# A fused attention, token-mixing and channel-mixing kernel: when the helper engines prepare the first weight pair, the Fourier folds and the side blocks

## The reference, cut to what matters

```python
# 1 attention with decay, blocks of 64, 2 batches x 8 heads, 768 x 64
intra = ((qb @ kb.T) * Dmask) @ vb;  inter = (qb * lam_pow) @ kv_state
out[:, :, sl] = intra + inter
kv_state = lam_block * kv_state + (kb * rev_pow).T @ vb
# 2 token mixing and a channel MLP, x: (2, 768, 512)
h  = np.maximum(x.T @ w_tok1, 0) @ w_tok2      # (512,768) @ (768,256) @ (256,768)
u  = x + h.T
x  = u + np.maximum(u @ w_ch1, 0) @ w_ch2      # 512 -> 1536 -> 512
# 3 real part of a 2-D Fourier transform, layer norm, a second MLP
u  = x + np.real(np.fft.fft(np.fft.fft(x, axis=1), axis=2))
un = (u - mean(u)) / np.sqrt(var(u) + 1e-6)
out = u + np.maximum(un @ w_ch1, 0) @ w_ch2    # 512 -> 2048 -> 512
```

## Time and profile before

| | |
|---|---|
| median of 3 runs (lowest, highest) | 600.6 us (599.02, 600.6) |
| the profiled execution, and its span | 599.33 us, 597.5 us |
| PE busy | 576.2 us, 96% of the span |
| DVE, ACT, POOL busy | 360.2, 263.0, 264.7 us (60%, 44%, 44%) |
| chain that ended last | PE 73%, DVE 10%, POOL 8%, ACT 3%, issue 3% |
| mean granted TensorE clock | 0.997 |

### The profile page before, as it was taken

How to read it: one execution, slowest core, us unless ns; L and a number is a source line. 1 busy time by engine, 2 the same in 40 slices (tenths; PEclk the granted TensorE clock), 3 DMA queues, 4 the chain that set the end, 5 groups by cost and what they waited for, 6 DMA issues and landing times.

```text
span 597.5 us, 9160 instructions
## 1 busy us (share of the span) xinstructions
PE 576.2 (96%) x3344; PEld 512.3 (86%) x3344; DVE 360.2 (60%) x675; ACT 263.0 (44%) x558; POOL 264.7 (44%) x306
## 2 busy tenths in 40 slices
PE   8999998899999989999989899999999999999997
PEld 6999886788889877989878779898888989999996
DVE  7887656657654587347786873477765544333323
ACT  6666134455643444333544443335453444443330
POOL 6884116555553473214457732044555233333311
PEclk9999999899999999999999999999999999999999
DMA  8791210322222101101121011021222211212242
GB/s 304 280 351 30 70 36 1 111 92 90 89 70 71 63 27 70 55 19 71 54 71 63 27 71 54 18 71 54 71 71 71 70 62 62 58 53 68 71 141 106
DMA packets 24125, 49.09 MB, mean 82 GB/s; under 512 B 2572, under 2 KB 3472, under 8 KB 24080
## 3 DMA queue, kind: packets, MB, share of 16 engines
q1 hardware_dynamic: 23360, 46.69, 23.6%
q0 software_dynamic: 576, 1.72, 1.0%
q10 hardware_dynamic: 144, 0.10, 0.1%
HBM read 45.35 MB, written 3.15 MB: 81 GB/s over the span
## 4 chain that ended last, share of the span: by engine, by line
PE 73%; DVE 10%; POOL 8%; ACT 3%; issue 3%; DMA 1%; SPq 1%; DVEq 0%; ACTq 0%; POOLq 0%
PE banks L1106 12%; PE banks L1107 11%; PE banks L1108 11%; PE banks L1333 9%; PE banks L1336 9%; PE banks L1335 9%; PE banks L1170 4%; DVE al L707 2%; POOL raw L346 2%; POOL tl L346 2%; PE banks L1130 2%; PE banks L1164 2%; POOL w2l L346 1%; DVE u L914 1%; DVE sums L707 1%
## 5 line engine op out<-in xcount | busy, mean ns | idle before, releaser
L346 POOL TENSOR_TENSOR w2l<-raw,w2h 128x512 fp32r<-128x512 f32 x56 | 77.4, 1383 | 178.4 <-ACT w2h L451 178.4
L1333 PE MATMUL banks<-th,al 128*128 128x384 f32 x392 | 132.9, 339 | 7.9 <-DVE snap L1028 5.0
L1335 PE MATMUL banks<-tl,ah 128*128 128x384 f32 x392 | 132.6, 338 | 0.0
L1336 PE MATMUL banks<-th,ah 128*128 128x384 f32 x392 | 132.4, 338 | 0.0
L451 ACT ACTIVATE snap<-banks 128x384 f32<-128x384 f32 x84 | 41.2, 490 | 133.4 <-PE banks L1336 133.3
L1028 DVE TENSOR_TENSOR snap<-banks,snap 128x384 f32<-128x384 f32 x84 | 46.3, 552 | 75.0 <-PE banks L1336 74.6
L1333 PEld LDWEIGHTS banks<-th,al 128*128 128x128 f32 x392 | 73.9, 189 | 17.5 <-DVE snap L1028 6.2
L707 DVE TENSOR_TENSOR al<-raw,ah 128x512 fp32r<-128x512 f32 (+1 forms) x112 | 83.5, 767 | 8.0 <-ACT ah L451 6.9
L1335 PEld LDWEIGHTS banks<-tl,ah 128*128 128x128 f32 x392 | 73.9, 189 | 6.0
L1336 PEld LDWEIGHTS banks<-th,ah 128*128 128x128 f32 x392 | 73.9, 189 | 0.0
L815 DVE SCALAR_TENSOR_TENSOR h0l<-snap,h0h 128x384 fp32r<-128x384 f32 x56 | 33.7, 602 | 63.7 <-ACT h0h L641 63.6
(11 more groups left out here) (176 smaller groups left out, 947.9 us busy)
## 6 DMA issues: line engine op xcount, KB each, us to landing
raw<-w1b_dram SPq DMA_DIRECT2D x16, 512.0 KB, 3.3
raw<-w2b_dram SPq DMA_DIRECT2D x32, 256.0 KB, 3.0
raw<-w1a_dram SPq DMA_DIRECT2D x12, 512.0 KB, 3.5
raw<-w2a_dram SPq DMA_DIRECT2D x24, 256.0 KB, 3.5
kTs<-kT_dram SPq DMA_DIRECT2D x8, 384.0 KB, 6.0
qTs<-qT_dram SPq DMA_DIRECT2D x8, 384.0 KB, 6.8
kns<-kn_dram SPq DMA_DIRECT2D x8, 384.0 KB, 7.3
vns<-vn_dram SPq DMA_DIRECT2D x8, 384.0 KB, 4.7
```

The lines of the kernel that those rows point to most:

```text
L346: return nc.gpsimd.tensor_tensor(o, i0, i1, ALU.subtract)
L1333: mm(o[:, 0:HALF], al[:, a, cols], th[b][:, t, k, :], start=start and k == 0, stop=False, skip_group_check=True)
L1335: mm(o[:, 0:HALF], ah[:, a, cols], tl[b][:, t, k, :], start=False, stop=False, skip_group_check=True)
L1336: last = mm(o[:, 0:HALF], ah[:, a, cols], th[b][:, t, k, :], start=False, stop=(k == 1), skip_group_check=True)
```

## The change

PE's and SP's instruction lists stay as they are. No instruction is added to or taken from the arithmetic; what changes is the order on ACT, DVE and POOL.

1. Token mixing. ACT makes the high parts of pair 0's weights after the second of the four `gh` tiles, not after the fourth; DVE makes their low parts after the second `gl`. POOL makes the combinations of pair 1 right after the down weights of pair 0, before the block sums' low parts (`tl`), and the clearing and loading of `e1raw` comes after these, still ahead of pair 1.
2. `combos` is cut in `combos12` and `combos34`; from pair 1 on `down_lo(p-1, 1)` stands between them, and in pair j = 1 of a Fourier chapter `fold_dif(.., 1)` too.
3. `fold_sum` is cut in `fold_even` and `fold_odd`. For the second tile the odd half comes after `h0l` and the `al` of the next pair; `fold_lo(.., 2)` moves behind the first `hidden_sum` of pair j = 2.
4. Side unit 2 is read by ACT ahead of the relu `h0h` and by DVE ahead of `h0l`; unit 3 by ACT ahead of the `up_second_hi`; the high parts of the block sums (`sums_hi`) come after that. In pair j = 3 side unit 0 (`dft_add` of the first tile) is read ahead of the first `h0l`.

The diff, without the lines that only rename and without a few context lines:

```diff
@@ -345,15 +345,26 @@
...
-def combos(p):
+def quarters():
+    return [raw1[:, i, k * 2 * L:(k + 1) * 2 * L] for i in range(2) for k in range(2)]
+def combos12(p):
+    if p >= NP:
+        return
     pool.wait_ge(s_w1, 16 * (p + 1))
...
         pool.wait_ge(blo_ready, p)
-    a11, a12, a21, a22 = [raw1[:, i, k * 2 * L:(k + 1) * 2 * L] for i in range(2) for k in range(2)]
+    a11, a12, a21, a22 = quarters()
     nc.gpsimd.tensor_tensor(sraw[:, RS1, :], a21, a22, ALU.add).then_inc(combo_step, 1)
...
     minus(sraw[:, RS2, :], sraw[:, RS1, :], a11).then_inc(combos_ready, 1)
+def combos34(p):
+    if p >= NP:
+        return
+    a11, a12, a21, a22 = quarters()
     minus(sraw[:, RS3, :], a11, a21)
@@ -400,28 +411,34 @@
...
-combos(0)
+combos12(0)
+combos34(0)
 down_lo(0, 0)
 down_lo(0, 1)
+combos12(1)
+combos34(1)
 for k, ready in ((T2, 1), (T3, 4), (T1, 4), (T4, 6)):
...
     minus(tl[0][:, k, :, :], source, f(th[0][:, k, :, :])).then_inc(sum_lo, 1 if k in (T2, T3) else 2)
+nc.gpsimd.memset(e1raw[:, :], 0.0).then_inc(pool_chain, 1)
+pool.wait_ge(pool_chain, steps_done + 1)
+for row in (slice(0, 1), slice(LO, LO + 1)):
+    pool.dma_start(e1raw[row, 0:NK1], e1).then_inc(s_erow, 16)
+    pool.dma_start(e1raw[row, W1PAD:W1PAD + NK2], alt).then_inc(s_erow, 16)
 for p in range(NP):
...
         root(ch - 1, 1)
-    if p + 1 < NP:
-        combos(p + 1)
-    if p == 0:
-        nc.gpsimd.memset(e1raw[:, :], 0.0).then_inc(pool_chain, 1)
-        pool.wait_ge(pool_chain, steps_done + 1)
-        for row in (slice(0, 1), slice(LO, LO + 1)):
-            pool.dma_start(e1raw[row, 0:NK1], e1).then_inc(s_erow, 16)
-            pool.dma_start(e1raw[row, W1PAD:W1PAD + NK2], alt).then_inc(s_erow, 16)
+    if p:
+        combos12(p + 1)
+    if fourier and j == 1:
+        fold_dif(ch - 1, 1)
     if p >= 2:
         down_lo(p - 1, 1)
+    if p:
+        combos34(p + 1)
     if ch == 0 and j < 4:
@@ -429,7 +446,6 @@
...
     if fourier and j == 1:
-        fold_dif(ch - 1, 1)
         fold_dif(ch - 1, 2)
@@ -558,11 +574,12 @@
...
     nc.scalar.activation(gh[:, m, :], bank[m][:, :], ACTF.Relu).then_inc(gh_ready, 1)
-up_first_hi(0)
-up_corner_hi(0)
-up_second_hi(0)
-down_hi(0, 0)
-down_hi(0, 1)
+    if m == KT - 1:
+        up_first_hi(0)
+        up_corner_hi(0)
+        up_second_hi(0)
+        down_hi(0, 0)
+        down_hi(0, 1)
@@ -624,7 +641,6 @@
...
         blocks2_hi(ch + 1, n, src)
-        sums_hi(ch + 1, n)
     elif what == "d1":
@@ -673,20 +689,25 @@
...
         fold_hi(ch - 1, 1)
+    side_hi(ch, j, 2)
     act.wait_ge(x_ready, 3 * p + 3)
...
     relu_hi(h0h[:, second], snap[:, 1, :])
-    side_hi(ch, j, 2)
+    side_hi(ch, j, 3)
     up_second_hi(p + 1)
+    units = SIDE[ch].get(j, EMPTY)
+    if units[3] and units[3][0] == "b2":
+        sums_hi(ch + 1, units[3][1])
     if fourier and j == 0:
...
         fold_hi(ch - 1, 2)
-    side_hi(ch, j, 3)
     side_hi(ch, j, 4)
     side_hi(ch, j, 5)
+    if units[5] and units[5][0] == "b2":
+        sums_hi(ch + 1, units[5][1])
     if p == 1:
@@ -823,10 +844,6 @@
...
-for m in range(B * KT):
-    dve.wait_ge(gh_ready, m + 1)
-    relu_lo(gl[:, m, :], bank[m][:, :], gh[:, m, :]).then_inc(gl_ready, 1)
 def up_first_lo(p):
@@ -880,14 +897,16 @@
...
-dve.wait_ge(rows_placed, 1)
-for n, t in enumerate((0, 3, 1, 4, 2, 5)):
-    token_out(0, t)
-    if n == 2:
+for m in range(B * KT):
+    dve.wait_ge(gh_ready, m + 1)
+    relu_lo(gl[:, m, :], bank[m][:, :], gh[:, m, :]).then_inc(gl_ready, 1)
+    if m == KT - 1:
         up_first_lo(0)
         up_corner_lo(0)
-    if n == 3:
         up_second_lo(0)
+dve.wait_ge(rows_placed, 1)
+for t in (0, 3, 1, 4, 2, 5):
+    token_out(0, t)
 token_out(1, 0)
@@ -913,7 +932,7 @@
...
-def fold_sum(b, a):
+def fold_even(b, a):
@@ -928,6 +947,9 @@
...
     nc.vector.tensor_copy(eo[b][:, i, FH:FH + 1], ssum[:, FH:FH + 1])
+def fold_odd(b, a):
+    n, i = NA * b + a, (NA * b + a) % 2
     dve.wait_ge(dif_ready, n + 1)
@@ -1033,10 +1055,15 @@
...
     if fourier and j == 1:
-        fold_sum(ch - 1, 0)
+        fold_even(ch - 1, 0)
+        fold_odd(ch - 1, 0)
     hidden_sum(p, 1, 0, 2)
     if fourier and j == 1:
-        fold_sum(ch - 1, 1)
+        fold_even(ch - 1, 1)
+    if fourier and j == 2:
+        fold_lo(ch - 1, 2)
+    if fourier and j == 3:
+        side_lo(ch, j, 0)
     if fourier and j == 4:
@@ -1050,8 +1077,11 @@
...
         minus(consts[n][2][:, :, 0:consts[n][4]], cview(n), f(consts[n][1][:, :, 0:consts[n][4]])).then_inc(cl_ready, 1)
-    side_lo(ch, j, 0)
+    if not (fourier and j == 3):
+        side_lo(ch, j, 0)
     side_lo(ch, j, 1)
+    if fourier and j == 1:
+        fold_odd(ch - 1, 1)
     if fourier and j == 4:
@@ -1069,15 +1099,16 @@
...
     hidden_sum(p, 3, 1, 7)
+    side_lo(ch, j, 2)
     hidden_lo(p, 4, h0l[:, second], snap[:, 1, :], h0h[:, second])
...
             add_out(ch - 1, t)
-    side_lo(ch, j, 2)
     side_lo(ch, j, 3)
     if fourier and j == 1:
-        fold_sum(ch - 1, 2)
+        fold_even(ch - 1, 2)
         fold_lo(ch - 1, 1)
+        fold_odd(ch - 1, 2)
     if fourier and j == 3:
@@ -1087,7 +1118,6 @@
...
         row_lo(ch - 1)
-        fold_lo(ch - 1, 2)
     if fourier and j == 4:
```

## The result

The changed kernel takes 590.43 us (median of 4 runs, 590.25 to 591.04), the kernel before on the same chip 600.53 (599.02 to 600.6). The ratio is 0.984 with a 95% interval of 0.9823 to 0.9857. The forecast was 589.5 with 585.2 to 593.2. The profiled execution took 590.4 us (span 588.6); that of before took 599.33, so 8.9 us of the 10.1 can be looked for between the two profiles.

What follows compares the result with a forecast made beforehand. PE, busy 96% of the span, was taken as the floor; gains in its gaps, 2.5 + 1.7 + 1.9 + 2.9 + 1.3 = 10.3 us, gave 589.0 from the profiled 599.33, stated as 589.5, range 585.2 to 593.2.

Steps and rivals of the forecast that it cites:

- pair 0, gaps: Waits at A22 (2.35) and S4 (1.79) shrink to 1.55 at S4, al held by POOL's last tl: 2.5 us won.
- pair 0, clock: Slow TensorE stretch behind pair 0's gaps, 103 to 113 us, goes as the clock stays up: 1.7 us won.
- folds, first batch: Pair 7: hidden_sum ends earlier though POOL holds up VectorE, so S4 comes at 220.15, 0.94 earlier; 0.95 us taken.
- folds, second batch: The first batch's fold gain of 0.95 us taken again; both batches 1.9 us, ends 0 and 5.
- pair 9, both batches: The 1.47 us wait for yp before the second q unit goes, twice: 2.9 us, ends 1.8 and 2.9.
- small waits: Third w2l wait won (0.5), other two nearly all given back at S4, transposes at 310.00 gain 0.7: together 1.3 us.
- a sign that it is wrong: The forecast is wrong if PE stands at an unlisted place, or al runs beside POOL in its usual 1.03.
- the same again 119.7 us later: Pair 7's waits, 1.83 us at S4 and 1.07 at the first Fourier unit, recur in the other batch.
- Rival 1: DVE and POOL don't get in each other's way at the new places: 14.5 us won, 585 us, chance 0.15.
- Rival 2: Stalls change their name: pair 7's hidden_sum no earlier, slow stretch stays; 6.7 us won, 592.6 us, chance 0.18.
- Rivals 3 and 4: 3: side unit 2 ahead of h0h stalls PE in twelve pairs, 604.6 us, chance 0.03; 4: gh late, 594 us, 0.04.
- rival 4: Token mixing: gh is late because ACT stands for the first weight load; 594 us, chance 0.04.

Runs made afterwards that it cites:

- e2_yp: Kernel before with only VectorE's Fourier sums of the first p unit moved ahead of h0l, in two pairs: 597.54 us, ratio 0.9952.
- e3_fold: Kernel before with the fold part alone (even and odd half apart, last fold_lo in the next pair): 598.43 us, ratio 0.9968.
- e1_tok: Kernel before with the token mixing part alone (pair 0's weights earlier, pair 1's combinations ahead of tl): 596.23 us, ratio 0.9941.
- e4_rest: Kernel before with the rest alone: side unit order, ScalarE's sums later, w2l ahead of two combinations outside the fold pairs: 599.42 us, ratio 0.9984.
- b1_order: Changed kernel; ahead of the second batch's folds, POOL's first w2l of the pair waits for VectorE's corner al: 592.03 us, ratio 0.9864.
- c4_sync: Changed kernel with b2_pair0's order and two POOL waits keeping w2l behind VectorE's al in the pair ahead of the second batch's folds: 587.42 us, ratio 0.9777.
- c1_clock: Kernel before with b2_pair0's edit, so S4's gap goes and A22's gap of 2.35 stays: 597.42 us, ratio 0.9944.
- b2_pair0: Changed kernel; in pair 0 VectorE does two token sums and the second hidden_sum ahead of pair 1's two al: 588.73 us, ratio 0.9819.
- c3_short: Changed kernel with b2_pair0's order; fold pairs' combinations 3 and 4 cut to 2 of 256 columns, values left out: 586.63 us, ratio 0.9763.
- b3_hoist: Changed kernel; in the two fold pairs VectorE does the second hidden_sum ahead of the two al and the odd half: 592.22 us, ratio 0.9877.

## Why the prediction came out right, point by point

| step | forecast | between the profiles |
|---|---|---|
| pair 0, gaps | 2.5 | 2.2 (4.14 before; 0.13 + 1.34 and 0.51 in pair 1 now) |
| pair 0, clock | 1.7 | 1.7 |
| folds, first batch | 0.95 | 0.96 (1.16 at S4 and 0.11 at the Fourier unit won, 0.31 lost at 230.85) |
| folds, second batch | 0.95 | -0.5 |
| pair 9, both batches | 2.9 | 2.96 |
| small waits | 1.3 | 1.3 |

The parts make 8.6 of the 8.9 us; the other 0.3 lies before pair 0 and in gaps under 0.12.

- **Pair 0** went by its mechanism: no wait at A22, al held up by the last tl, S4 at 1.34 (1.55 said). The 0.51 in pair 1 was not foreseen. The forecast named PE standing at a place outside as a sign that it is wrong, and this sign came: the late weight load of pair 1 took 5.1 us to land, where the working had 3.5 for such a load.
- **The clock** held, as said. What was missed is that its price varies. The profiled one of before had a mean clock of 0.997; 41 of the 64 had 0.994 or less. In e2_yp's profile, with the same two gaps, both stretches behind them are slow:

```profile
109.00:113.00 4.00, 3.18 (x9) 2.99 (x10) 2.68 (x6) 1.47 (x4) 2.92 (x5) 0.51 0.18 29
113.00:117.00 4.00, 4.00 (x15) 3.69 (x15) 1.52 (x2) 1.48 (x3) 0.00 (x0) 0.64 0.95 340
```

  That is 4 x 0.49 + 4 x 0.36 = 3.4 us instead of 1.7. It may be why the medians are 10.1 apart and the profiles 8.9, but the times bear it out only in part: of the 64 executions the 23 with 0.996 or 0.997 average 599.9 us and the 41 others 600.7, which is 0.8 and not 1.7. So there is luck in the number. Measured from profile to profile, as it was worked out, the gain was 1.4 us too large (589.0 against 590.4), which is the second batch's folds; the step up to 589.5 for the median made the miss 0.9.
- **Folds.** The step that failed is "the same again 119.7 us later". The first batch did what was said: ssum ended at 211.1 (215.1 said, 4.1 us later in the old time), even half 212.5, h0l 213.5, each held up by the POOL operation named. That the batch then came to 0.96 is two errors that cancel: S4 won 1.16, and moving fold_lo, said to cost nothing as "the unit waits for both", goes with 0.31 more lost at the second Fourier product (0.80 in e3_fold, 0.5 in e1_tok, e2_yp and before). The second batch isn't its copy. The w2l wait of PE before it is gone, and POOL's w2l and VectorE's corner al met 0.05 us apart in the pair ahead of the folds, at 317.2. From the first A11 of the fold pair to ssum it is 204.72 to 206.66 in the first batch and 320.70 to 324.18 in the second: VectorE was 1.5 us later relative to PE. e3_fold (no miss), e4_rest (the miss without folds), b1_order and c4_sync (part of it and most of it taken out) show it. The two terms of the sum, folds and small waits, weren't independent.
- **Pair 9** went to 0.1 us.
- **Small waits** have the right sum by the wrong parts. The three w2l waits gave 1.0 instead of 0.5, as S4 took back 0.3 in pair 11 and 0.3 in its twin, and the third is gone; the transposes gave 0.35 of the 0.7 said, and the main one still waits 0.82 for VectorE's tl.
- **Rivals.** Rival 1 (no contention) is out: al took 2.39 for two. Rival 2 was right for one fold of two. Rivals 3 and 4 didn't come: no wait for unit 2, and gh on time, but with 1.07 us to spare, so rival 4 was nearer than its 0.04 said.
- **Sums.** Two slips in the working had no effect: the places that it lists add up to 17.3 us, not 20, and the upper end of the folds is 5.8 by its own terms, not 5.

The Trainium skill's page "TensorE: Matmul & The Clock Gate", section "A second HAM failure mode: psum-queue depth-cycling", tells of a kernel in which frequent short idles between groups of matmuls made the clock go up and down; by this the slow stretch would have stayed. The changed kernel's trace disagrees there, with gaps of 0.13 and 1.34 at a clock of 1.00. In c1_clock, one gap of 2.35 went with the lower clock in three executions of seven.

## What to carry to other kernels

When PE is the floor, list its gaps in order of time, put a releaser and a price to each, and look for a second row of the same time on the engines that release it: in the places shown here, a VectorE operation with two SBUF inputs at twice its usual length had a POOL operation beside it, and the list of PE's waits doesn't name that. Give such a place operations that read PSUM, or move POOL's operations into its idle time, rather than move the wait. When a gap is gone, look at the trace for what else went with it: a part of b2_pair0's gain came by a weight load that landed earlier. And don't double a gain because a stage occurs twice: look at who arrives how early in each, since a gain elsewhere shifts one engine against another, and 0.05 us can decide over 1.1.

## What the hardware showed that was not expected

- The hold-up went by order of arrival and lasted a whole operation: a corner al (0.42 alone) that came 0.05 us behind a w2l of 1.29 took 1.52; the one that began 0.50 us ahead of it (b1_order) took 0.42. With starts 0.01 us apart by the trace, POOL first, it was POOL that was held up: w2l took 1.59 and al 0.42 (c3_short).
- A load of 512 KB took 5.0 to 5.7 us to land when one of 579 KB from POOL's queue had been issued 0.8 to 1.4 us ahead of it, and 3.3 to 4.2 when the two were issued within 0.13 us of each other (c1_clock among them).
- The clock didn't act alike in equal executions: with a gap of 2.35 alone, 4 of 7 had a mean clock of 1.00. In the second batch it fell behind a gap of 2.78 (e4_rest) and behind one of 2.01 with one of 1.00 two us later (b3_hoist), where 1.83 had left it at 1.00.
